# One core, attention and two feed-forward layers: four final results turned, copied and stored one by one, and the first groups of layer 2 reordered

## The reference

```python
qn = q / (norm(q, axis=1) + 1e-6);  kn = k / (norm(k, axis=1) + 1e-6)      # q, k, v: 6016 x 256, f32
s  = kn.T @ qn / tau                                                        # 256 x 256
a  = softmax(s, axis=-1)
x  = v @ a                                                                  # 6016 x 256
h  = x @ w_in1;   y1 = where(h > 0, h, exp(min(h, 0)) - 1) @ w_out1         # d_ff = 2048, layer 1
h2 = y1 @ w_in2;  out = (h2 * sigmoid(h2)) @ w_out2                         # d_ff = 2048, layer 2
```

## Time and profile before

| | before |
|---|---|
| median of 3 runs | 1014.74 us (1014.49 to 1014.88) |
| profiled execution: time | 1014.23 us |
| profiled execution: span | 1012.4 us |
| TensorE busy | 1004.1 us, 99% of the span, 4750 matmuls |
| weight loads busy | 893.9 us |
| VectorE busy | 782.0 us |
| ScalarE busy | 576.6 us |
| GpSimd busy | 10.2 us |

### The profile page before, as it was taken

One profiled execution on the slowest core, in us unless ns is written; L12 is line 12 of the kernel. 1 busy time (PEld: TensorE's weight loads), 2 busy tenths in 40 slices (PEclk: granted clock), 3 DMA queues, 4 the chain that ended last, 5 costly groups with the idle time before them and its releaser, 6 DMA issues.

```text
span 1012.4 us, 13274 instructions
## 1 busy us (share of the span) xinstructions
PE 1004.1 (99%) x4750; PEld 893.9 (88%) x4750; DVE 782.0 (77%) x1107; ACT 576.6 (57%) x915; POOL 10.2 (1%) x11
## 2 busy tenths in 40 slices
PE   9999999999999999999999999999999999999997
PEld 8888888888888888889999788888888888888997
DVE  7789878778777777777775766877877886887886
ACT  6676545555545444454445656656666665655664
POOL 0300000000000000000000000000000000000000
PEclk9999999999999999999999999999999999999999
DMA  9902313333111021124103325236237236234342
GB/s 355 369 15 73 110 63 94 114 89 109 79 21 49 15 63 42 19 59 168 42 37 146 110 73 192 92 89 236 73 95 236 85 93 204 107 93 129 110 104 84
DMA packets 114166, 109.77 MB, mean 108 GB/s; under 512 B 89024, under 2 KB 96320, under 8 KB 111552
## 3 DMA queue, kind: packets, MB, share of 16 engines
q1 hardware_dynamic: 113728, 108.58, 33.0%
q10 hardware_dynamic: 384, 0.49, 0.1%
HBM read 83.23 MB, written 25.82 MB: 108 GB/s over the span
## 4 chain that ended last, share of the span: by engine, by line
PE 98%; ACT 1%; issue 1%; DVE 1%; DVEq 0%; POOL 0%; POOLq 0%
PE bank L1105 73%; PE bank L1252 20%; PE bank L1115 4%; PE bank L1133 0%; ACT g_pair L750 0%; PE bank L1284 0%; DVE m_tile L1083 0%; ACT g_pair_parts L757 0%; ACT g_pair_parts L764 0%; PE bank L1292 0%; DVE g_forms L978 0%; PE bank L1148 0%; DVE out_tile L1095 0%; PE bank L1154 0%; ACT early_scores L669 0%
## 5 line engine op out<-in xcount | busy, mean ns | idle before, releaser
L1105 PE MATMUL bank<-x_parts,w_in_parts 128*128 128x512 f32 (+1 forms) x1152 | 274.6, 375 | 1.5 <-ACT g_pair L750 1.5
L1105 PE MATMUL bank<-g_parts,w_out_parts 128*128 128x512 f32 (+1 forms) x1152 | 274.8, 375 | 0.0
L1105 PE MATMUL bank<-xT_parts,a_w_in 128*128 128x512 f32 (+1 forms) x1152 | 274.3, 375 | 0.0
L727 ACT ACTIVATE g_raw<-bank 128x512 f32<-128x512 f32 (+1 forms) x192 | 112.9, 588 | 234.5 <-PE bank L1105 222.8
L1105 PEld LDWEIGHTS bank<-x_parts,w_in_parts 128*128 128x128 f32 x1152 | 215.6, 189 | 30.6 <-ACT g_pair L750 2.9
L1105 PEld LDWEIGHTS bank<-xT_parts,a_w_in 128*128 128x128 f32 x1152 | 217.7, 189 | 26.0
L1105 PEld LDWEIGHTS bank<-g_parts,w_out_parts 128*128 128x128 f32 x1152 | 217.7, 189 | 25.8
L1252 PE MATMUL bank<-g_pair_parts,w_forms 128*128 128x512 f32 (+1 forms) x987 | 239.3, 375 | 0.0
L1252 PEld LDWEIGHTS bank<-g_pair_parts,w_forms 128*128 128x128 f32 x987 | 186.5, 189 | 22.1
L750 ACT ACTIVATE g_pair<-bank 128x512 f32<-128x512 f32 (+1 forms) x192 | 112.9, 588 | 133.9 <-PE bank L1105 126.8
L947 DVE TENSOR_SCALAR g_raw<-g_raw 128x512 f32<-128x512 f32 (+1 forms) x192 | 80.1, 417 | 93.1 <-ACT g_raw L727 92.3
(11 more groups left out here) (84 smaller groups left out, 357.9 us busy)
## 6 DMA issues: line engine op xcount, KB each, us to landing
w_forms<-w_forms SPq DMA_DIRECT2D x48, 896.0 KB, 4.6
y_parts<-y1T_parts SPq DMA_DIRECT2D x10, 1024.0 KB, 3.9
x_parts<-y_parts SPq DMA_DIRECT2D x10, 1024.0 KB, 8.4
w_forms<-w_out_forms SPq DMA_DIRECT2D x8, 896.0 KB, 4.7
early_qk<-q SPq DMA_DIRECT2D x23, 256.0 KB, 7.8
early_qk<-k SPq DMA_DIRECT2D x22, 256.0 KB, 8.1
out<-out_tile SPq DMA_DIRECT2D x40, 128.0 KB, 2.7
v_in<-v SPq DMA_DIRECT2D x36, 128.0 KB, 3.4
```

The source lines that it names most:

```text
L727: act.activation(g_sb[:, f % 2, 0:ph.n], h_ps[f % N_H][:, 0:ph.n], ACT.Exp).then_inc(u_act, 1)
L1105: mm = pe.matmul(dst, lhsT, rhs, start=first and n == 0, stop=last and n == len(todo) - 1)
```

## The change

It edits three places of layer 2. (1) `FIRST_H`: up groups 4 to 7 of the first tile take banks 4, 0, 4, 5 in place of 0, 4, 5, 0. (2) In the third pair of the first tile, ScalarE does each of the four silus ahead of the high-part copy that stood before it. (3) At the end, `LAST_PRODUCTS` has M6 ahead of M3; each of the four results gets a bank of its own (`row_banks[n]`), is copied whole (ScalarE the first three, VectorE the last) and stored on its own as 448 rows of 128 columns (512 B pieces): the first three by the sync queue, each after its copy, the last by ScalarE's queue.

```diff
-LAST_PRODUCTS = (M1, M2, M3, M6, M7, M5, M4)
+LAST_PRODUCTS = (M1, M2, M6, M3, M7, M5, M4)
-FIRST_H = (0, 1, 2, 3, 0, 4, 5, 0)
+FIRST_H = (0, 1, 2, 3, 4, 0, 4, 5)
...
-        LAST_HALVES = (1, 0)
-        row_banks = (m_banks[M1], m_banks[M6]), (bank[0], m_banks[M2])
-        def out_rows(a, i):
-            return o_sb[0:LAST_P, a, :, :, :].rearrange("p g c i -> p (g c i)")[:, 2 * C * i:2 * C * (i + 1)]
-        def last_store(eng, a, i):
-            eng.wait_ge(l_rows[a][i], 1)
-            first = N - (2 - a) * T_LAST + 2 * i * LAST_P
-            eng.dma_start(out[first:first + 2 * LAST_P, :].rearrange("(w x) c -> x w c", w=2),
-                          out_rows(a, i).rearrange("p (w c) -> p w c", w=2)).then_inc(d_out, 16)
+        row_banks = bank[0], m_banks[M1], m_banks[M2], m_banks[M6]
+        def out_rows(turn):
+            c, a = turn
+            return o_sb[0:LAST_P, a, :, :, :].rearrange("p g c i -> p (g c i)")[:, c * 4 * P:(c + 1) * 4 * P]
+        def last_store(eng, turn):
+            c, a = turn
+            first = N - (2 - a) * T_LAST
+            eng.dma_start(out[first:first + T_LAST, c * P:(c + 1) * P].rearrange("(w x) c -> x w c", w=4),
+                          out_rows(turn).rearrange("p (w c) -> p w c", w=4)).then_inc(d_out, 16)
...
-            last_store(sp, LAST_HALVES[0], 0)
-            last_store(sp, LAST_HALVES[0], 1)
-            last_store(sp, LAST_HALVES[1], 1)
+            for n in range(len(LAST_TURNS) - 1):
+                sp.wait_ge(l_rows_act, n + 1)
+                last_store(sp, LAST_TURNS[n])
...
+                        silu_first = u is TWO[0] and k == LAG_PAIRS
+                        if silu_first:
+                            silu(u, k, i)
                         if back:
                             (sums_hi if i < 2 else plain_hi)(*back, i % 2)
                         if u.before and (k, i) in K_ACT_COPY:
                             m_copy(u.before, M_ACT[K_ACT_COPY.index((k, i))])
-                        silu(u, k, i)
+                        if not silu_first:
+                            silu(u, k, i)
...
-            for a in LAST_HALVES:
-                act.wait_ge(l_turn, LAST_HALVES.index(a) + 3)
-                act.activation(out_rows(a, 0), row_banks[a][0][0:LAST_P, :], ACT.Copy).then_inc(l_rows[a][0], 1)
-            last_store(act, LAST_HALVES[1], 0)
+            for n in range(len(LAST_TURNS) - 1):
+                act.wait_ge(l_turn, n + 1)
+                act.activation(out_rows(LAST_TURNS[n]), row_banks[n][0:LAST_P, :], ACT.Copy).then_inc(l_rows_act, 1)
+            act.wait_ge(l_rows, 1)
+            last_store(act, LAST_TURNS[-1])
...
-            for a in LAST_HALVES:
-                dve.wait_ge(l_turn, LAST_HALVES.index(a) + 3)
-                dve.tensor_copy(out_rows(a, 1), row_banks[a][1][0:LAST_P, :]).then_inc(l_rows[a][1], 1)
+            dve.wait_ge(l_turn, len(LAST_TURNS))
+            dve.tensor_copy(out_rows(LAST_TURNS[-1]), row_banks[-1][0:LAST_P, :]).then_inc(l_rows, 1)
...
-                    mm = pe.transpose(row_banks[a][w // 2][0:LAST_P, (w % 2 * CB + c) * P:(w % 2 * CB + c + 1) * P],
+                    mm = pe.transpose(row_banks[n][0:LAST_P, w * P:(w + 1) * P],
```

More of the change, by code:

```diff
@@ L254, in build @@
         l_turn = sem("last_c_turned")
-        l_rows = [[sem(f"last_rows{a}{i}") for i in range(2)] for a in range(2)]
+        l_rows = sem("last_rows_by_dve")
+        l_rows_act = sem("last_rows_by_act")
         c_out = sem("c_summed")
```

## The result

| | before | with the change |
|---|---|---|
| median | 1014.74 us (15 runs, 1014.12 to 1015.12) | 1012.03 us (15 runs, 1011.45 to 1012.78) |
| ratio | | 0.9974, 95% interval 0.9966 to 0.9982 |
| profiled execution: time, span | 1014.23, 1012.4 us | 1011.59, 1009.8 us |
| TensorE busy | 1004.1 us | 1004.0 us |

The change takes 2.7 us off, 0.27%. The forecast was 1012.2 us, within 1011.4 to 1013.2. The work is the same; two seams are shorter. Two distances within one trace measure them, and do not depend on when the stretch begins: the **head**, from the start of the run of 30 up matmuls that begins with group 3 to the start of group 12, and the **tail**, from the first of the last pair's 21 products to the end of the span.

What follows compares the result with a forecast made beforehand. TensorE was taken as the bound, leaving only seams: banks 0, silus first -1.75, M6 ahead of M3 +0.08, four stores -0.90, sum -2.57, say -2.55. From 1014.74 that gave 1012.2 us, range 1011.4 to 1013.2.

Steps and rivals of the forecast that it cites:

- Rival (c): In the head, the wait shifts to groups 10 to 12, so only 1.1 is gained there: 1012.8 us; chance 0.13.
- the model: At the end, landing estimated as issue, 2.4 us alone and 1.06 queueing: the old last store lands at 11.86.
- The 0.1 us added for the pieces: At the end, a lone final store in 512 B pieces was put at 2.5 us to land, against 2.4 before.
- the line between 128 B and 1 KB: At the final stores, a 512 B piece's cost taken on a straight line between those two sizes' costs: 26.8 ns.
- Rival (b): At the final stores, 512 B pieces run at full rate, 23.3 ns; tail gives 1.10, sum -2.85: 1011.9 us; chance 0.22.
- (a): The forecast itself: both seams, head and end, gain, sum -2.55: 1012.2 us; chance 0.50.
- (d): At the final stores, 512 B pieces cost as much as four of 128 B; sum -0.55: 1014.2 us; chance 0.10.
- (e): At the final stores, half-row pieces in flight hinder each other; at 60 ns the sum is +0.7: 1015.5 us; chance 0.03.

Runs made afterwards that it cites:

- the second trace: The changed kernel, unaltered, run once more on the same chip as a kernel combining further edits: 1012.03 us, ratio 0.9973 against the kernel before.

## Why the prediction was right

**The head** came out by its own steps. Group 9 without a wait, groups 10 and 11 each with 0.10 us for late weights, the high part of the second sums held by VectorE but in time: all in the rows, -1.78 against -1.75. The order alone does it and the banks do nothing, each shown by a run of its own. The reason given for the banks' nought, a wait that counts two silus too many, is shown by the run that shortened it: 0.43 us, as worked out. Rival (c), a gain of only 1.1, is out: no wait of TensorE over the 0.10 for late weights stands at groups 10 to 12.

**M6 ahead of M3** was priced at +0.08 and measures +0.11: the products stretch by 0.26 (0.25 forecast), the last sum ends 1.91 behind the last product (1.9 forecast). This part of the change works against it. The old order ends the last sum 0.11 us earlier, M7 ahead of M3 0.41; neither gain is seen in the tail beyond its scatter.

**The four stores** were priced at -0.82 together with that, and the tail gave -1.00 (-1.12 in the second trace). The issue times were right: the last store 7.83 after the first product, where 1008.15 - 1000.36 = 7.79 was forecast. The errors lay in the landing. Before, the model gave 11.86 where the trace had 12.0; taking its own 11.86 as the start costs the forecast 0.14 of the 0.18 us that it was short. With the change it gave 2.5 alone and 0.39 of queueing, 2.89; measured are 2.3 and 0.5, 2.8, so two errors partly cancel. The 0.1 us added for the pieces was wrong, though the packet's own time on an engine was not: 26.9 ns, where the line between 128 B and 1 KB said 26.8. Rival (b) so was half right: it had the landing of a lone store nearer (2.4), but not the packet's time, 23.3 ns. Its queueing of 0.21 adds up to 0.19 from its own terms, which moves it by 0.02 only. The times alone could not have told (a) from (b): -2.71 lies midway between their -2.55 and -2.85; the packet's time decides. Rivals (d) and (e), slow pieces, are out: 26.9 ns against the 48 that (d) takes and the 53 at which (e) begins to be slower.

**The sum** was -2.55 and is -2.64 between the profiled executions and -2.71 between the medians. The closeness of the first is partly luck: head and tail together gave -2.78, and layer 2 happened to begin 0.18 us later in the trace of the changed kernel (549.41 against 549.23), in a part that the change doesn't touch. The ratio's interval, 0.9966 to 0.9982, still takes in 0.998, so that the gain is over 0.2% is likely but not shown.

## What to carry to other kernels

Where one engine is busy for 99% of the span, what is left lies in the seams: list its waits, and at each ask which instruction the late one is queued behind on its own engine, and then what the next ones would be queued behind; here the order of four pairs on ScalarE was worth two thirds of the gain. The new banks freed nothing until the wait's count was lowered with them. At the end of a program, look at when the first store goes, not only the last: here 0.4 us won on the last issue gave 0.10 and 0.15 in two traces, no more than the scatter, while starting the stores over 2.3 us and not over 0.9 took 0.8 off the slowest landing.

## What the runs showed of the hardware

- A lone store of 224 KB lands in 2.3 us, in 224 pieces of 1 KB and in 448 of 512 B alike. With four stores in flight, a packet of 512 B on ScalarE's queue takes 26.9 ns on an engine and one of 1 KB 46.5; in the lone stores they take 27.5 (0.095 x 8.4 x 16 / 464) and 49.8 (0.089 x 8.4 x 16 / 240). One of 128 B takes 12.1. The Trainium skill ("DMA: Bandwidth & Descriptors", Specifications) puts line rate at 512 B and above. The landing agrees with it; the packet's time by itself is 10% above half of the 1 KB packet's in the lone stores (27.5 against 24.9) and 16% in the others (26.9 against 23.3).
- Of the 3.6 us that the last store took before, 1.3 were queueing behind the three others.
- The same code up to group 3 of layer 2 reaches it at 549.09 to 550.39 us in the profiled executions here (the kernel before with one store, and the one with the shorter wait). That is more than any single part of this change, save the silus' order, is worth, so parts were compared by distances within a trace; these repeat within 0.01 us for the head and 0.17 for the tail.
